# High and low halves of the first product's weights interleaved value by value, in a fused convolution and two-layer MLP kernel

## The reference

```python
w = softmax(weight_gen, axis=-1)                    # 7 taps for each of 8 heads, 24 features a head
att[b, s, h] = sum(w[b, s, h, k] * x_pad[b, s + k, h] for k in range(7))   # causal window of 7 rows
x = att.reshape(8192, 192)
h = np.maximum(x @ moe_w_in, 0.0)
x = h * h @ moe_w_out                               # layer one
h = x @ moe2_w_in
g = h * np.clip(h + 3.0, 0.0, 6.0) / 6.0
out = g @ moe2_w_out                                # layer two
```

## Time and profile before

| | |
|---|---|
| time, median of 2 runs | 1126.93 us (1126.91 to 1126.94) |
| span of the profiled execution, first to last instruction | 1125.2 us |
| the median of the runs less that span | 1.7 us |
| PE (matmuls) | 1119.4 us busy, 99%, 9940 instructions |
| PEld (weight loads) | 1082.5 us busy, 96%, 9940 instructions |
| DVE | 906.8 us busy, 81%, 985 instructions |
| ACT | 668.8 us busy, 59%, 747 instructions |

### The profile page before, as it was taken

One profiled execution on the slowest core, in us unless ns is written; L12 is line 12 of the kernel. 1 busy time (PEld: TensorE's weight loads), 2 busy tenths in 40 slices (PEclk: granted clock), 3 DMA queues, 4 the chain that ended last, 5 costly groups with the idle time before them and its releaser, 6 DMA issues.

```text
span 1125.2 us, 25509 instructions
## 1 busy us (share of the span) xinstructions
PE 1119.4 (99%) x9940; PEld 1082.5 (96%) x9940; DVE 906.8 (81%) x985; ACT 668.8 (59%) x747; POOL 3.1 (0%) x10
## 2 busy tenths in 40 slices
PE   9999999999999999999999999999999999999998
PEld 8998999999999999999999999999999999999997
DVE  8788796987969789697887978879698797976665
ACT  7986556565565655645556555555655556456554
POOL 1000000000000000000000000000000000000000
PEclk9999999999999999999999999999999999999999
DMA  7221002020110201103020020200202002010001
GB/s 214 86 66 36 6 16 63 4 74 7 30 48 3 75 6 57 25 0 77 4 66 15 0 77 4 70 11 8 69 4 73 8 17 59 0 40 4 1 16 29
DMA packets 79302, 41.28 MB, mean 37 GB/s; under 512 B 56172, under 2 KB 72300, under 8 KB 79272
## 3 DMA queue, kind: packets, MB, share of 16 engines
q1 hardware_dynamic: 79144, 40.64, 13.9%
q10 hardware_dynamic: 128, 0.22, 0.1%
HBM read 29.42 MB, written 11.40 MB: 36 GB/s over the span
## 4 chain that ended last, share of the span: by engine, by line
PE 99%; DVE 0%; DMA 0%; ACT 0%; issue 0%; DVEq 0%
PE h_ps L1131 46%; PE y_ps L1141 31%; PE y_ps L1149 21%; PE h_ps L988 0%; DMA wraw<-in_weight_gen_dram 0%; PE y_ps L1099 0%; PE y_ps L988 0%; PE y_ps L1272 0%; PE h_ps L1099 0%; PE y_ps L1253 0%; DVE prod L721 0%; PE y_ps L1254 0%; PE y_ps L1259 0%; PE y_ps L1256 0%; PE h_ps L1089 0%
## 5 line engine op out<-in xcount | busy, mean ns | idle before, releaser
L1131 PE MATMUL h_ps<-xt,win 64*128 64x512 f32 x4552 | 1026.4, 386 | 0.0
L1131 PEld LDWEIGHTS h_ps<-xt,win 64*128 64x128 f32 x4552 | 801.3, 184 | 14.9
L1141 PE MATMUL y_ps<-hid_hi,wout 64*128 64x512 f32 x2032 | 542.5, 386 | 0.0
L503 ACT ACTIVATE hid_hi<-hid 128x1024 fp32r<-128x1024 f32 x240 | 254.7, 1061 | 328.9 <-DVE hid L822 166.0
L831 DVE TENSOR_TENSOR hid_lo<-hid,hid_hi 128x1024 fp32r<-128x1024 f32 x253 | 309.5, 1223 | 147.6 <-ACT hid_hi L503 141.5
L1141 PEld LDWEIGHTS y_ps<-hid_hi,wout 64*128 64x128 f32 x2032 | 373.3, 184 | 7.1 <-PE y_ps L1141 0.3
L1141 PE MATMUL y_ps<-hid_lo,wout 64*128 64x512 f32 x1016 | 311.6, 386 | 0.0
L1149 PE MATMUL y_ps<-hid_hi,wout 64*128 64x512 f32 x1016 | 311.4, 386 | 0.0
L1149 PE MATMUL y_ps<-hid_lo,wout 64*128 64x512 f32 x1016 | 311.3, 386 | 0.0
L1141 PEld LDWEIGHTS y_ps<-hid_lo,wout 64*128 64x128 f32 x1016 | 186.8, 184 | 4.0 <-DVE hid_lo L806 0.3
L1149 PEld LDWEIGHTS y_ps<-hid_hi,wout 64*128 64x128 f32 x1016 | 186.9, 184 | 3.7 <-PE y_ps L1149 0.3
(11 more groups left out here) (116 smaller groups left out, 358.1 us busy)
## 6 DMA issues: line engine op xcount, KB each, us to landing
xwin<-in_x_dram SPq DMA_DIRECT2D x14, 960.0 KB, 5.9
by_feature<-stage SPq DMA_DIRECT2D x52, 96.0 KB, 2.0
out_dram<-outs SPq DMA_DIRECT2D x240, 16.0 KB, 1.5
out_dram<-outs SPq DMA_DIRECT2D x240, 8.0 KB, 1.4
stage<-by_feature SPq DMA_DIRECT2D x13, 256.0 KB, 3.0
stage<-in_moe_w_out_dram SPq DMA_DIRECT2D x8, 384.0 KB, 3.6
stage<-in_moe_w_in_dram SPq DMA_DIRECT2D x8, 256.0 KB, 3.7
stage<-in_moe_w_in_dram SPq DMA_DIRECT2D x16, 128.0 KB, 3.7
```

Of the source, the lines that this page charges most:

```text
L503: act.activation(hi, hid[:, slot], ACT.Copy).then_inc(hi_done, 1)
L1131: return pe.matmul(h_ps[:, s % 2, t, :], win[layer][r, wn, cols], src[r, xn, :], start=bool(rows) and n in (0, SHORT), stop=not rows and n ...
L1141: return pe.matmul(ps[:, 0, :], wout[layer][r, tile, w_cols], src, start=bool(rows) and s == 0 and n == 0, stop=not rows and s == STEPS - ...
```

## The change

For each layer `win` becomes two tensors, `win_main` and `win_rest`, each [128, 2048, 2]: high and low half of one weight lie side by side, 4 bytes each. What was a run of 128 values is now every second value, a step of 8 bytes, both for TensorE's loads and for the writes of ScalarE and VectorE that make the halves. The bytes in all are the same. Between `win_main0` and `win_rest0` lie 128 unused bytes (`ahead`), and 128 more behind `win_rest0` (`behind`), so `win_rest0` lies 128 bytes further in each partition and `win_main1`, `win_rest1`, `wout` and all tensors after them 256 bytes further. `last_hi` and `last_lo` take the first and second 1024 values of `win_main0` and `win_rest0` as flat memory. The order of instructions on each engine, their shapes and their waits stay as they were.

```diff
-        win = [sb(f"win{n}", [P, 4, FF], fp32r) for n in range(2)]
+        win_main, win_rest = [], []
+        for n in range(2):
+            win_main.append(sb(f"win_main{n}", [P, FF, 2], fp32r))
+            if n == 0:
+                ahead = sb("ahead", [P, Q], fp32r)
+            win_rest.append(sb(f"win_rest{n}", [P, FF, 2], fp32r))
+            if n == 0:
+                behind = sb("behind", [P, Q], fp32r)
+
+        def win(layer, w):
+
+            return (win_main, win_rest)[w // 2][layer][:, :, w % 2]
+
...
-        last_hi, last_lo = [[win[0][:, 2 * n + m, 0:PAIR * N].rearrange("p (t n) -> p t n", t=PAIR) for m in range(2)]
-                            for n in range(2)]
+        last_hi, last_lo = [[(win_main, win_rest)[n][0][:, :, :].rearrange("p f a -> p (f a)")[:, m * PAIR * N:(m + 1) * PAIR * N]
+                             .rearrange("p (t n) -> p t n", t=PAIR) for m in range(2)] for n in range(2)]
...
-                hi = win[layer][:, 2 * rest, cols]
+                hi = win(layer, 2 * rest)[:, cols]
...
-                return [(win[layer][:, 2 * rest + 1, part * QC:(part + 1) * QC], raw, hi)]
+                return [(win(layer, 2 * rest + 1)[:, part * QC:(part + 1) * QC], raw, hi)]
...
-                return pe.matmul(sums_of(s, 0)[:, t, :], win[0][r, w, cols], xt[1][r, x, :], start=start, stop=stop,
+                return pe.matmul(sums_of(s, 0)[:, t, :], win(0, w)[r, cols], xt[1][r, x, :], start=start, stop=stop,
...
-                return pe.matmul(h_ps[:, s % 2, t, :], win[layer][r, wn, cols], src[r, xn, :],
+                return pe.matmul(h_ps[:, s % 2, t, :], win(layer, wn)[r, cols], src[r, xn, :],
...
-                    return pe.matmul(h_ps[:, (STEPS - 1) % 2, 0, :], win[1][REST:P, w, tile * P:(tile + 1) * P],
+                    return pe.matmul(h_ps[:, (STEPS - 1) % 2, 0, :], win(1, w)[REST:P, tile * P:(tile + 1) * P],
```

## The result

The changed kernel takes 1144.51 us (1144.26 to 1144.76, 2 runs), the kernel before 1126.93. The ratio is 1.0155, with a 95% interval of 1.0136 to 1.0174: 17.6 us slower, clear of noise, and inside the 2% that I called "same". The profiled execution spans 1142.5 us, 17.3 us more than before. The forecast of no change by 2% holds, and so does the range of 1118 to 1190. The forecast time of 1127.0 us is 17.5 us too low, and the measured time lies outside the likeliest case's own range, 1120 to 1133.

What follows compares the result with a forecast made beforehand. The prediction took TensorE's matmul count times pace as the bound. Its terms summed 0 + 0 + 0, leaving the median of 1126.93 us, so it forecast 1127.0 us, range 1118 to 1190.

Steps and rivals of the forecast that it cites:

- same: Whole kernel: time changes by no more than 2% (22.5 us) either way; chance 0.68.
- likeliest case: Whole kernel: the layout changes nothing the chip notices, 1127.0 us, own range 1120 to 1133; chance 0.68.
- the collisions: Rival that the kernel gets slower by collisions, up to which the range reaches, 1190 us; chance 0.14.
- What bounds the kernel: Whole kernel: TensorE (PE) bounds it, 99% of the chain; time is the number of matmuls times their pace.
- Part 1, the step of 8 bytes: Loads with `win` reading a value every 8 bytes: taken as 0; 0 to 23 us if the reading rate halves.
- the slot is as long as the slower of the two: Loop: two matmuls, one per row group, form a slot of 0.2267 us whose length the slower one sets.
- the count of 4554: Pairs of matmuls holding one with `win`, 253 steps of 18; each ns longer costs 4.55 us.
- a gain on `win` alone gives 0: Loop: each pair with `win` also holds a `wout` matmul, so speeding up `win` alone gains 0.
- the faster rival: Rival that the whole kernel gets faster by over 2%; chance 0.11.
- Part 2, the moved addresses: `win_rest` of layer one 128 bytes further, all behind it 256: taken as 0; 128 bytes not in the trace.
- Part 3, the splits: ACT's and DVE's splits of weights writing with a step, mostly beside PE's work: taken as 0.
- The 3 us kept in the range: Allowance of 3 us for splits of weights not covered, before and in the first sums.

Runs made afterwards that it cites:

- e1: The changed kernel without the two unused stretches of 128 bytes, halves interleaved, all tensors at the old addresses; 1143.63 us against 1127.03 for the kernel before, ratio 1.0148.
- e3: All four kinds of weights of a layer interleaved in one tensor, a step of 16 bytes, no unused stretches; 1157.47 us, ratio 1.0272 to the kernel before.
- e10: Kernel before, but products with `win` load one value 128 times in place of 128 values; 1136.85 us, ratio 1.0086.
- e2: The changed kernel with high and low halves one behind the other, keeping the two unused stretches; 1138.23 us, ratio 1.0099 to the kernel before.
- e9: Kernel before with 240 unused bytes behind `wout`, which move the moving operands by 256 bytes; 1127.03 us, ratio 1.0001.
- e8: Kernel before with 16 unused bytes behind `wout`, which move the moving operands by 32 bytes; 1158.79 us, ratio 1.0280.
- e6: Kernel before with 128 unused bytes ahead of `win`, so all tensors move and distances stay; 1126.99 us, ratio 1.0000.
- e5: Kernel before with 128 unused bytes behind `wout`, so moving operands lie 128 bytes further and weights stay; 1157.58 us, ratio 1.0270.

## Why the prediction was right, and where it was not

The range and "same" held. The reasoning behind them holds in part, and that "same" held is in part luck. All three terms of the sum were 0, and the first measured 16.6 us. Its price for one product, 6.67 ns, is above the 4.9 ns from which the prediction called the kernel slower; the whole stayed under 2% only because that price is paid about ten times a step and not 18. The range held because it reached up to the collisions. The prediction also took 2% for about what a measurement can tell from no change; the intervals here are some 0.2% wide each way, and 1.5% stands clear of them.

*What bounds the kernel*: right. PE's pace was all of it (99% of the chain before and after), at the same clock.

*Part 1, the step of 8 bytes*: taken as 0, measured at 16.6 us (e1), inside the 0 to 23 us that I had kept as a bound, but for another reason than the one given there. The load does not take a second 0.11 us: its record grew by 6 ns. Had it done so, most of it would have been covered, as argued: in e3 it grew by 122 ns, and the products by at most 13. What failed is the sentence that "the slot is as long as the slower of the two" and with it the count of 4554. In e1 the two row groups do not wait for each other slot by slot: eight intervals took 1.86 us on one and 1.82 on the other. They have paces of their own, and since each has `win` for half of a step, the price is paid about ten times a step and not 18 times. By slots, the measured 6.67 ns would have been 4554 x 6.67 = 30 us, out of "same". The same mistake was in "a gain on `win` alone gives 0": with separate paces a gain would have been a gain. No layout here gave one, so that is argued and not shown.

*The rival with collisions*, up to which the range reaches, was nearest to what the runs show: a price in each product with `win`, steady through the loop. No run shows the term from which its 1190 us were worked out; the runs show in its place 6.67 ns, ten times in 253 steps (e1). A price that doubles with the bytes that a load spreads over falls with e3 (128 stretches of 16 bytes in a load, 231 to 240 ns) and e10 (one stretch, 226 to 234 ns). For the faster rival no run shows anything: no step's mean is below 226.7 ns a product.

*Part 2, the moved addresses*: taken as 0. In the change it is 0.9 us (1144.51 - 1143.63, measured at different times), on contiguous weights 11.2 us (e2). The reading of the earlier trace rows was right for what it could show: 256 bytes do nothing (e9, and `win_main0` in e2). 128 bytes were not in the trace, as said, and 0 was wrong for them: in e2 the intervals grow by up to 14 ns, and those of products next to `win_rest` grow too.

*Part 3, the splits*: DVE 0, ACT 50 ns each, 0.06 us in the first sums. Right. The 3 us kept in the range rest on a cost that no run shows at a step of 8 bytes; at 16 bytes DVE took 424 ns more for a split and ACT 526 (e3).

What stays open is where the 6.7 ns arise. That the pace depends on the distance between weights and moving operand is shown: with loads recorded alike at 184 ns, moving operands 32 bytes further raise a product from 226.7 to 233.3 ns (e8), and moving all tensors together by 128 bytes does nothing (e6, 1126.99 us). Why it does is not shown, nor why 64 bytes cost a third of what 32, 128 and 192 cost (2.2 ns against 6.7), nor why a step of 8 bytes costs 6.67 ns at the distance of before.

## What to carry to other kernels

Where TensorE is the bound and every matmul has its load, look at the distance in a partition between weights and moving operand: a small tensor of 16 to 192 bytes allocated between them cost 0.9 to 2.8% here, and what shows it in the profile is starts 2.2 to 6.7 ns further apart, with loads recorded at 184 or 185 ns as before. Count in what a tensor really takes: one of 16 bytes moved all behind it by 32 (e8), one of 240 by 256 (e9). Distances of 0 and 256 bytes beyond that of before were the ones without a loss. Keep weights contiguous (226.7 ns a product), or at the least with two fp32 values in each 16 bytes: that cost 1.5% here (e1), one value in each 16 bytes 2.7% (e3). And when two row groups run beside each other, count what each of them has to do by itself; a price on one kind of product was paid ten times a step here, by the row group that had it, and not in all 18 slots (e1).

## What was not expected of the hardware

- The pace of a 64x512 product with a load of its own took three values in steady state: 226.7, 228.9 and 233.3 ns, by the distance between weights and moving operand; 0 and 256 bytes gave the first, 64 the second, 32, 128 and 192 the third. Shifting all tensors by 128 bytes gave 1126.99 us against 1127.01.
- Mixed distances are worse than their share: 8 of a step's 38 products at 128 bytes cost 93 ns a step (e2), all 38 of them 126 (e5: 4432.2 - 4306.7). Why is not shown.
- A load with a step of 16 bytes is recorded at 306 ns in place of 184, and products beside such loads are still only 0.23 to 0.24 us apart.
- Loading one value 128 times costs more than loading 128 values: two of three products with `win` at 233 or 234 ns in place of 226.7 (e10).
